# Second MoE layer: the gather of tile 2 goes ahead of tile 0's scale lookup, and the scales are stored by partition from ScalarE's queue

## The reference

```
logits = x @ w_gate
e_idx  = argmax(logits)
gate_w = softmax(logits)[e_idx]
eom    = sigmoid(x @ w_output_gate)[e_idx]
for e in experts:
    h  = relu(x[mask] @ w1[e])
    ye = h @ w2[e]
    out[mask] = gate_w * eom * ye
```

## Time and profile before

| | |
|---|---|
| median of 3 runs | 944.36 us (942.32 to 945.37) |
| the profiled execution, its own time | 948.46 us |
| its span | 946.7 us |
| mean granted TensorE clock | 0.975 |
| PE busy | 889.7 us, 94% |
| DVE busy | 371.2 us, 39% |
| ACT busy | 265.4 us, 28% |
| POOL busy | 157.7 us, 17% |

### The profile page before, as it was taken

One profiled execution on the slowest core, in us unless ns is written; L12 is line 12 of the kernel. 1 busy time (PEld: TensorE's weight loads), 2 busy tenths in 40 slices (PEclk: granted clock), 3 DMA queues, 4 the chain that ended last, 5 costly groups with the idle time before them and its releaser, 6 DMA issues.

```text
span 946.7 us, 21670 instructions
## 1 busy us (share of the span) xinstructions
PE 889.7 (94%) x8176; PEld 801.0 (85%) x8177; DVE 371.2 (39%) x814; ACT 265.4 (28%) x484; POOL 157.7 (17%) x208
## 2 busy tenths in 40 slices
PE   8898999999999999999999999997659999999994
PEld 6797899989899898999989899996548888888883
DVE  5675885313223131322314222246534222624421
ACT  4563454222122222222222122124123111513321
POOL 5773302500000000000000000000122222332321
PEclk9998999999999999999999999999679999999997
DMA  9984743300000100000010010005511112415110
GB/s 246 247 215 135 226 129 118 84 23 23 13 33 0 44 0 11 33 11 33 0 44 0 11 33 0 23 1 200 196 28 44 44 44 85 170 49 194 49 34 18
DMA packets 64207, 68.46 MB, mean 72 GB/s; under 512 B 32414, under 2 KB 48926, under 8 KB 64160
## 3 DMA queue, kind: packets, MB, share of 16 engines
q1 hardware_dynamic: 57600, 45.21, 16.0%
q0 software_dynamic: 6560, 22.56, 7.6%
HBM read 54.11 MB, written 14.69 MB: 73 GB/s over the span
## 4 chain that ended last, share of the span: by engine, by line
PE 90%; DMA 3%; issue 2%; DVE 2%; SPq 1%; ACT 0%; POOL 0%; POOLq 0%; DVEq 0%
PE bank L1067 33%; PE bank L1088 16%; PE bank L1210 11%; PE bank L1191 10%; PE bank L959 4%; PE bank L1036 4%; PE bank L983 4%; PE bank L1203 2%; PE bank L1104 2%; DMA scale_rows<-r_scale 1%; PE bank L1019 1%; PE bank L1097 1%; PE bank L1174 1%; DMA e_w<-w 1%; DMA k_sb<-kT 1%
## 5 line engine op out<-in xcount | busy, mean ns | idle before, releaser
L746 DVE TENSOR_TENSOR prod<-silu,bank 128x256 f32<-128x256 f32 x108 | 45.5, 421 | 249.8 <-ACT silu L538 249.8
L1067 PE MATMUL bank<-x_hi,wg_hi 128*128 128x256 f32 x432 | 125.3, 290 | 0.0
L1067 PE MATMUL bank<-x_hi,wv_hi 128*128 128x256 f32 x432 | 122.3, 283 | 0.0
L1067 PE MATMUL bank<-x_lo,wv_hi 128*128 128x256 f32 x432 | 122.3, 283 | 0.0
L1067 PE MATMUL bank<-x_hi,wv_lo 128*128 128x256 f32 x432 | 122.2, 283 | 0.0
L1067 PE MATMUL bank<-x_hi,wg_lo 128*128 128x256 f32 x432 | 122.2, 283 | 0.0
L1067 PE MATMUL bank<-x_lo,wg_hi 128*128 128x256 f32 x432 | 122.1, 283 | 0.0
L538 ACT ACTIVATE silu<-bank 128x256 f32<-128x256 f32 x108 | 41.5, 384 | 253.0 <-PE bank L1067 253.0
L1088 PE MATMUL bank<-wo_hi,h_hi 128*128 128x512 f32 x216 | 85.8, 397 | 0.0
L1088 PE MATMUL bank<-wo_hi,h_lo 128*128 128x512 f32 x216 | 84.3, 390 | 0.0
L1088 PE MATMUL bank<-wo_lo,h_hi 128*128 128x512 f32 x216 | 84.2, 390 | 0.0
(11 more groups left out here) (188 smaller groups left out, 1608.3 us busy)
## 6 DMA issues: line engine op xcount, KB each, us to landing
e_w<-w SPq DMA_DIRECT2D x32, 512.0 KB, 4.9
stage<-w_out POOLq DMA_DIRECT2D x16, 384.0 KB, 4.1
x_in<-x_rows SPq DMA_DIRECT2D x9, 512.0 KB, 3.6
y_rows<-y_sb SPq DMA_DIRECT2D x18, 256.0 KB, 2.0
k_sb<-kT SPq DMA_DIRECT2D x16, 256.0 KB, 5.8
v_sb<-v SPq DMA_DIRECT2D x16, 256.0 KB, 5.1
q_sb<-qT SPq DMA_DIRECT2D x16, 256.0 KB, 3.1
x_rows<-x_sb SPq DMA_DIRECT2D x16, 256.0 KB, 3.3
```

The source lines that it names most:

```text
L746: dve.tensor_tensor(prod[:, c % 2, :], silu[:, c % 2, :], bank[2 + c % 2][:, 0:GT], ALU.mult).then_inc(prod_ready, 1)
L1067: mm = pe.matmul(acc[:, 0:GT], w[:, k, cols], x[:, k, :], start=(k == 0 and i == 0), stop=(k == KC - 1 and i == 2))
```

## The change

It has four edits.

1. On POOL, tile 0 is taken out of the loop, and the gather of tile 2 (`gather_ahead(0)`) stands in front of the wait for the store of the scales and of tile 0's lookup. In the loop, now from tile 1, the order stays.
2. The store leaves SP's queue and goes to ACT's, behind `rows_high(0)` and in front of ACT's wait for `tab_ready`. It is no longer in token order: `scale_rows` takes partition after partition, so that each of 128 partitions writes 18 numbers (72 bytes) in one piece.
3. Since token n now lies at (n mod 128) * 18 + n / 128, DVE makes `scale_at` from `place_rows` with three instructions of 128 x 144 at the end of `scales()`.
4. In each tile POOL copies a second column, of `scale_at` to `scale_row`, and looks the scales up with it; `row_out` serves the scatter alone.

```diff
-            sp.wait_ge(scale_ready, 1)
-            sp.dma_start(scale_rows.rearrange("(t p) o -> p (t o)", p=P), r_scale[:],
-                         allow_slow_non_contiguous=True).then_inc(scale_out, 16)
...
-            pool.wait_ge(scale_out, 16)
             tiles = pool.value_load(table[0:1, T_TILES:T_TILES + 1], min_val=1, max_val=SLOTS)
-            with pool.Fori(0, tiles) as t:
+
+            def gather_ahead(t):
+                pool.wait_ge(xt_done, alone(pool, t + 2))
+                gather(t + 2, pool.value_load(table[0:1, bass.ds(t + (T_COL + 2), 1)], min_val=0, max_val=PLACES - 1))
+
+            def tile(t):
                 col = pool.value_load(table[0:1, bass.ds(t + T_COL, 1)], min_val=0, max_val=PLACES - 1)
                 pool.tensor_copy(row_out[:], place_rows[:, bass.ds(col, 1)]).then_inc(ro_ready, 1)
+                pool.tensor_copy(scale_row[:], scale_at[:, bass.ds(col, 1)]).then_inc(sr_ready, 1)
                 pool.wait_ge(ro_ready, alone(pool, t + 1))
+                pool.wait_ge(sr_ready, alone(pool, t + 1))
                 pool.indirect_dma_start(scale_in[:], None, scale_rows,
-                                        bass.IndirectOffsetOnAxis(ap=row_out[:, 0:1], axis=0),
+                                        bass.IndirectOffsetOnAxis(ap=scale_row[:, 0:1], axis=0),
                                         bounds_check=NT - 1, oob_is_err=False).then_inc(sc_in, 16)
-                pool.wait_ge(xt_done, alone(pool, t + 2))
-                ahead = pool.value_load(table[0:1, bass.ds(t + (T_COL + 2), 1)], min_val=0, max_val=PLACES - 1)
-                gather(t + 2, ahead)
+                if not isinstance(t, int):
+                    gather_ahead(t)
                 pool.wait_ge(o_ready, alone(pool, t + 2))
...
+            gather_ahead(0)
+            pool.wait_ge(scale_at_ready, 1)
+            pool.wait_ge(scale_out, 16)
+            tile(0)
+            with pool.Fori(1, tiles) as t:
+                tile(t)
...
             rows_high(0)
+            act.wait_ge(scale_ready, 1)
+            act.dma_start(scale_rows.rearrange("(p t) o -> p (t o)", p=P), r_scale[:]).then_inc(scale_out, 16)
             act.wait_ge(tab_ready, 1)
...
                 dve.reciprocal(r_scale[:], r_s1[:]).then_inc(scale_ready, 1)
+                then(dve.tensor_scalar(at_part[:], place_rows[:], P - 1, None, ALU.bitwise_and),
+                     dve.tensor_scalar(at_tile[:], place_rows[:], 7, None, ALU.logical_shift_right))
+                dve.scalar_tensor_tensor(out=scale_at[:], in0=at_part[:], scalar=float(TILES), in1=at_tile[:],
+                                         op0=ALU.mult, op1=ALU.add).then_inc(scale_at_ready, 1)
```

More of the change, by code:

```diff
@@ L157, in build @@
         place_rows = sb("place_rows", [P, PLACES], U32)
+        scale_at = sb("scale_at", [P, PLACES], U32)
+        at_tile, at_part = (sb(n, [P, PLACES], U32) for n in ("at_tile", "at_part"))
+        scale_row = sb("scale_row", [P, 1], U32)
         pl_none, pl_row = (sb(n, [P, PLACES]) for n in ("pl_none", "pl_row"))
@@ L215, in build @@
         scale_out = sem("scale_out")
+        scale_at_ready = sem("scale_at_ready")
+        sr_ready = sem("sr_ready")
         rows_ready = sem("rows_ready")
```

## The result

The changed kernel took 933.27 us (median of 4 runs, 931.92 to 936.66) against 943.63 us of the kernel before (median of 4 runs that day): ratio 0.9891, 95% interval 0.9872 to 0.991. Two more comparisons, each with a profile of its own, gave 0.9927 (0.9905 to 0.995) and 0.9904 (0.9879 to 0.9928). The forecast was 934.3 us, with a range of 931.6 to 939.0.

A forecast was written before the change was run, and what follows sets the result against it. PE bounds the kernel, except for one 9.07 us wait in the expert layer behind the store and gather. Saving 10.08 us with nothing taken back, 944.36 becomes 934.3 us, range 931.6 to 939.0.

The forecast's parts named there:

- The waits: Expert layer, tile 1: store waits behind SP's queue, gather behind the store; PE idles 9.07 us before turn_rows(2).
- the scales still late: Rival: store lands as late as now, at 696.7; only 1.7 us saved, 942.7 us; chance 0.08 (or nothing changes).
- edit 1: Gather of tile 2 ahead on POOL: starts at 683.6, lands between 686.9 and 691.2, removing PE's 9.07 us wait.
- Tile 1: Layer2 of tile 1 starts at 696.45 after 0.7 us idle; tile 2 begins at 702.46 instead of 712.54, 10.08 us saved.
- has nothing random in it: Said of the profiled stretch around tile 1, so the same 10.1 us was taken off the median of 944.36.
- the margin for `turn_rows(3)`: Tile 1: gather(3) issued at 704.3 or a little later, landing at 707.8; PE wants it at 708.38, 0.6 us to spare.
- The store's landing: Store issued by ACT lands between 674.4 and 687.9, from almost nothing to 13.49 us; said to decide nothing.
- Edit 4: POOL's second copy, 0.18 us plus a wait in each tile; tile 10 has 0.8 us to spare, the copy takes 0.2.
- POOL is too late: Rival in tile 1: missed by up to 2 us, 935 to 937 (0.09); fully blocked by `e_lo`, 939.0 (0.05).
- The slow case: Rival: the store holds ACT's queue, delaying tile 0's relu; held until 696.74 gives 954.0 us; chance 0.03.
- Edit 3: Three DVE instructions before `hT_lo` of tile 0, about 0.3 us each; 1 us under a cover of 5 costs nothing.

The follow-up runs named there:

- one wide copy: Changed kernel with place_rows and scale_at interleaved, so one POOL copy of two columns replaces two; ratio to the kernel before 0.9922.
- the three experiments with the store in token order: New POOL order, one copy, 2304-piece store: behind SP's weight loads (ratio to the kernel before 0.9991), on ACT's queue (0.9938), ahead of SP's loads (0.9943).
- only the store: Changed kernel but with POOL's old order, tile 0's lookup ahead of the gather of tile 2; ratio to the kernel before 0.9901.
- SP first by partition: Changed kernel with its 128-piece store issued by SP ahead of the eight weight loads instead of by ACT; ratio to the kernel before 0.992.
- the third copy: Changed kernel with one more POOL column copy in each tile, between row_out and scale_row; run once, stretch 270.9 us, no ratio.
- the order with `row_out` behind the gather: Changed kernel with the wait for the scatter and the copy of row_out moved behind gather_ahead; ratio to the kernel before 0.9886, repeat 0.9898.

## Why the prediction was right, and where it was not

**The waits.** Two in a row, the store behind SP's queue and the gather behind the store: shown, by the runs with one of them removed. They are not worth the same. With the gather alone early the stretch fell by 1.1 us; with the store alone early all of tile 1's gain. I had priced the first case as a rival (the scales still late, 1.7 us). Tile 2 came 1.68 us earlier, but that this agrees is luck: layer2 of tile 1 began 31.93 us after `turn_rows(0)` instead of 34.85, 2.9 us earlier and not 1.7, and from there to tile 2 it took 8.38 us at the low clock and not 7.14. And I wrote of edit 1 as if it were needed, and had not worked out the second case.

**Tile 1.** 10.08 us forecast; 9.49, 9.05 and 8.86 in the three executions of the changed kernel (41.99 less 32.50, 32.94 and 33.13). The steps behind the sum stand: the gather issued 2.5 us behind the start of `turn_rows(1)`, `o_sb` right behind `e_lo`, PE idle 0.5 where I had 0.7. The lookup followed the gather after 2.2 us where I had 3.6, which nothing waited for. Most of the missing 0.6 to 1.2 us lies in tile 0, which I had taken as fixed ("has nothing random in it"): `turn_rows(1)` started 10.95, 11.44 and 11.62 us after `turn_rows(0)`, instead of 10.59. In the first of these PE waited 0.23 us for the rows of tile 1. The store beside that gather isn't the reason, since with only POOL's order changed, and the store as late as before, PE waited 0.26 us there; why is open. In the other two tile 0 begins with 11 and 12 matmuls of 0.63 us, the length at a granted clock of 0.50, where the kernel before has 7. That is scatter: over all kernels the number goes from 5 to 12. In the margin for `turn_rows(3)` the terms add up to a gather at 704.4 and 0.5 us to spare, where I wrote 704.3 and 0.6; PE didn't wait there in any run.

**The store's landing.** Between almost nothing and 13.49 us, said to decide nothing: 7.2 to 7.8 us, and it decided nothing. But the upper bound was not a bound. Beside the loads 2304 pieces took 20.0 us, and that would have decided. The row of 13.49 us was of a store issued behind the loads.

The Trainium skill says in "DMA: Bandwidth & Descriptors", section "Rules for kernel authors", that a last dimension which isn't contiguous is lowered to one descriptor for each element, and advises to rearrange. The runs agree: on ACT's queue the store in token order is 2320 packets and the one by partition 144, each 16 more than its pieces. As to time, of which the sentence says nothing, 2304 pieces took 13.0 to 20.0 us and 128 pieces 3.0 to 7.8 us.

**Edit 4.** This is the step that failed: "the copy takes 0.2 of it", of the 0.8 us to spare in tile 10. I added a copy's own length to the chain and did not ask what each copy meets. The runs together show the price of each. In tile 10, by the number of POOL copies in front of the lookup that began behind the start of `e_lo`:

| copies that met `e_lo` | runs | start of `e_lo` to the gather's issue | PE idle before `turn_rows` |
|---|---|---|---|
| none | the kernel before, one wide copy | 3.26, 3.28 us | 0 |
| one | the three experiments with the store in token order | 4.40 to 4.41 us | 0.27 to 0.35 us |
| two | three of the changed kernel, only the store, SP first by partition | 5.53 to 5.55 us | 1.22 to 1.39 us |
| three | the third copy | 6.63 us | 2.38 us |

Each copy that meets `e_lo` puts the gather back by 1.1 us, about one `e_lo`. Two put it back by 2.3 us, less the margin of 0.8 that is 1.5, near the idle 1.22 to 1.39 us. The trace that I had read has its copy at 808.96, 0.21 us ahead of `e_lo`, and that was chance. In the three runs with one copy it began 0.35 to 0.95 us behind, so the kernel before may lose 0.3 us there in other executions too. The timeline of all engines in tile 10 with only POOL's order changed:

```profile
803.30 4.63 DVE L811 TENSOR_TENSOR e_lo<-e_w,e_hi  x4 [1.68 <-ACT e_hi L568]
...
803.73 0.84 POOL L481 COPY row_out<-place_rows 128x1 uint32 x1 [7.99 <-issue]
...
811.32 0.65 PE L1183 MATMUL bank<-ident,xg 128*128 128x128 f32 x4 [0.35 <-DMA xg<-y_rows,row_in]
```

Of the rival "POOL is too late" I had the price of one blocked copy right, 1.16 us, but had put it in tile 1, on the evidence of POOL's DMA issues beside `e_lo`; in the runs those took mostly 1.1 to 1.5 us instead of 1.03, at most 1.98, and never one `e_lo` more for each of a chain of them.

Here the Trainium skill's "SBUF — State Buffer", section "Who interferes with whom", was right where I had gone by the rows: the second to come waits for the whole instruction. The copies of 0.84, 1.13, 1.19 and 1.20 us agree with that, and the one that began 0.02 us ahead of `e_lo` and took 0.17 does too. What it says of the whole instruction it says of DVE's two-port modes; the runs show it for a `tensor_tensor` too. I had also read the section too broadly: it says that a `tensor_tensor` with both inputs in SBUF, which `e_lo` is, gets in the way of GpSimd's reads, and that it did not stall the DMAs. So a stretched DMA issue was no evidence on the copies.

**The slow case.** ACT's queue was not held by the store: issue in 0.35 to 0.40 us. The relu of tile 0 came 7.56 us after `turn_rows(0)` (670.12), where it was 7.57 before, and 7.16 us after it even with the store of 2304 pieces. It came after 8.29 us in the two executions with 11 and 12 slow matmuls, where ACT waited for PE. Edit 3, three DVE instructions of 0.42, 0.17 and 0.31 us, is covered as forecast.

The sum for the expert layer was therefore 10.1 - 0.6 - 1.4 = 8.1 us, where I had 10.1. The medians fell by 10.4 us, and that this meets the forecast so closely is luck: the traces account for 8.1, and the ratios of the other two comparisons say 6.9 and 9.0.

## What to carry to other kernels

Where an engine waits for work that doesn't need what it waits for, follow both chains: here moving the gather alone gained 1.1 us of the 8.1, since PE wanted the scales right behind the rows, and the early scales alone freed the gather as well. Lay a small DRAM tensor out so that each partition writes one piece, and pay with index arithmetic; thousands of 4-byte writes are slow themselves and hold up the transfers around them. When an instruction is added to a chain with a thin margin, look up what runs beside it at that moment on the other engines. Where one waits for the other, as POOL's copies did for DVE's `e_lo`, its cost is the length of that neighbour, not its own. And a margin read from one trace can be there by chance; look at the same place in a second one.

## What the runs showed of the hardware

**A POOL copy waits for the DVE instruction that runs.** `e_lo` has two inputs in SBUF and takes 1.16 us; copies of 128x1 that come while one runs end about 0.1 us behind it, one `e_lo` for each copy (0.84, 1.19 and 1.20 us for three in a row), while DVE is hardly slowed: four in a row take 4.63 to 4.68 us in the expert layer of every run.

**A short idle time of PE sometimes lowers the clock.** Before tile 1's `turn_h` PE idled 1.75 to 1.90 us in all runs but one (5.60 us), with no lower clock behind it in the kernel before, which I had taken for a rule. With the wide copy the matmuls after 1.89 us were at the low level. Stretches of that run: start:end, length, busy time of PE, PEld, DVE, ACT and POOL, granted clock, DMA share, GB/s:

```profile
686.00:688.00 2.00, 0.47 (x3) 0.05 (x1) 2.00 (x3) 2.00 (x3) 0.00 (x0) 1.00 0.00 0
688.00:690.00 2.00, 1.64 (x7) 1.42 (x8) 2.00 (x3) 0.91 (x2) 0.00 (x0) 0.73 0.01 4
690.00:692.00 2.00, 2.00 (x8) 1.54 (x7) 1.63 (x3) 0.00 (x0) 0.46 (x1) 0.50 0.00 0
```

The run of the order with `row_out` behind the gather shows it after 1.90 us and its repeat doesn't after 1.88; the run with three copies doesn't after 1.90; with SP first by partition it is there after 1.87. What decides stays open. From tile 1's first matmul to tile 2's it took 15.95 to 15.97 us with it and, in the other runs with early scales, 15.02 to 15.16 us without, so it cost 0.9 us, as much as the effects that I was measuring.

**The scatter lands late where the next expert's loads begin.** In tile 10 POOL stood 7.35 to 8.5 us behind the scatter of 256 KB instead of the 2.7 to 3.1 us of the tiles without loads, in every kernel in which POOL waits for it. The eight loads begin about 1.4 us before the scatter there; no run leaves them out, so that they are the cause isn't shown. The late landing makes the thin margin there, and it is why taking it out of the chain pays.
